# Batch 0 of a three-stage fp32 pipeline: three token tiles turned later, and unread products in the waits of the transform

## The reference, cut to what matters

```python
X = np.fft.fft(x, axis=1); X = np.fft.fft(X, axis=2)
u = x + np.real(X)                                   # x: (4, 768, 320)
mu = np.mean(u, axis=-1, keepdims=True)
var = np.mean((u - mu) ** 2, axis=-1, keepdims=True)
un = (u - mu) / np.sqrt(var + 1e-06)
out = u + np.maximum(un @ w_ch1, 0.0) @ w_ch2        # w_ch1: (320, 1280), w_ch2: (1280, 320)
```

## Time and profile before

| | |
|---|---|
| median of 3 runs | 972.84 us |
| lowest, highest | 966.74, 973.04 us |
| the profiled execution, its device time | 971.5 us |
| its span, first to last instruction | 969.7 us |
| mean granted PE clock | 0.935 |
| instructions | 29104 |
| PE busy in the span | 846.5 us (87%) |

### The profile page before, as it was taken

How to read it: one execution, slowest core, us unless ns; L and a number is a source line. 1 busy time by engine, 2 the same in 40 slices (tenths; PEclk the granted TensorE clock), 3 DMA queues, 4 the chain that set the end, 5 groups by cost and what they waited for, 6 DMA issues and landing times.

```text
span 969.7 us, 29104 instructions
## 1 busy us (share of the span) xinstructions
PE 846.5 (87%) x12612; PEld 810.1 (84%) x12612; DVE 595.4 (61%) x1187; ACT 386.8 (40%) x732; POOL 173.4 (18%) x191
## 2 busy tenths in 40 slices
PE   1738987997987997979879769999999999999998
PEld 1638876886886997978769669999999999999998
DVE  7692996785775685470446654776557573675622
ACT  1325315524424524525156334642446324562311
POOL 2016154182173074222100000000000000000000
PEclk9859997997997998996979979999999999999999
DMA  9601726476377186156682010000200001000000
GB/s 327 210 31 66 220 73 204 143 245 210 97 229 229 51 263 209 67 140 178 235 326 88 1 49 14 8 1 1 70 22 1 1 22 49 22 1 1 21 21 21
DMA packets 56095, 100.96 MB, mean 104 GB/s; under 512 B 28241, under 2 KB 40274, under 8 KB 51538
## 3 DMA queue, kind: packets, MB, share of 16 engines
q1 hardware_dynamic: 55970, 99.11, 31.0%
HBM read 76.40 MB, written 22.70 MB: 102 GB/s over the span
## 4 chain that ended last, share of the span: by engine, by line
PE 40%; DVE 8%; issue 1%; ACT 1%; DVEq 0%; POOL 0%; ACTq 0%
PE psum L1351 18%; PE psum L1411 9%; PE psum L1377 8%; PE psum L1431 2%; DVE stats L1234 1%; PE psum L1447 1%; DVE res L1244 1%; DVE hid L1180 1%; DVE res L1225 1%; DVE tok L1236 1%; PE psum L1342 1%; DVE cv L1257 1%; DVE res L1226 1%; DVE cv L1255 1%; DVE gs L1175 0%
## 5 line engine op out<-in xcount | busy, mean ns | idle before, releaser
L1351 PE MATMUL psum<-xn,w 128*128 128x384 f32 x640 | 126.6, 341 | 3.4 <-issue 3.4
L1351 PEld LDWEIGHTS psum<-xn,w 128*128 128x128 f32 x640 | 111.5, 190 | 4.4 <-issue 4.4
L1351 PE MATMUL psum<-xs,w 128*128 128x384 f32 x512 | 97.2, 343 | 10.2 <-PEq L1547 7.9
L1351 PEld LDWEIGHTS psum<-xs,w 128*128 128x128 f32 x512 | 91.6, 194 | 10.6 <-issue 10.6
L1377 PE MATMUL psum<-w,gs 128*128 128x320 f32 x576 | 89.9, 310 | 4.2 <-DVE gs L1175 4.1
L1377 PEld LDWEIGHTS psum<-w,gs 128*128 128x128 f32 x576 | 86.3, 188 | 5.7 <-DVE gs L1175 5.7
L552 DVE TENSOR_TENSOR score<-bank,mask 128x512 f32<-128x512 f32 x48 | 32.4, 688 | 71.0 <-PE bank L778 70.2
L535 DVE TENSOR_TENSOR inv<-inv,outer 128x31 f32<-128x31 f32 (+15 forms) x186 | 64.9, 349 | 6.4
L753 PE MATMUL bank<-inv_t,rhs 128*80 128x128 f32 x384 | 59.7, 329 | 9.2 <-POOL inv_t L452 4.6
L753 PEld LDWEIGHTS bank<-inv_t,rhs 128*80 128x80 f32 x384 | 56.2, 189 | 10.3 <-issue 9.8
L533 DVE TENSOR_TENSOR outer<-low,inv 128x31 f32<-128x31 f32 (+15 forms) x186 | 62.0, 334 | 4.3
(11 more groups left out here) (127 smaller groups left out, 1647.3 us busy)
## 6 DMA issues: line engine op xcount, KB each, us to landing
kb<-in_kb SPq DMA_DIRECT2D x24, 512.0 KB, 6.1
rt<-in_rt SPq DMA_DIRECT2D x12, 1024.0 KB, 7.2
w_in<-in_tables SPq DMA_DIRECT2D x13, 499.0 KB, 3.6
high_scratch<-w_in SPq DMA_DIRECT2D x13, 499.0 KB, 3.9
low_scratch<-w_in SPq DMA_DIRECT2D x13, 499.0 KB, 4.7
w_in<-in_w SPq DMA_DIRECT2D x6, 1040.5 KB, 5.1
at<-in_a SPq DMA_DIRECT2D x6, 1024.0 KB, 4.9
zt<-in_vt SPq DMA_DIRECT2D x12, 512.0 KB, 8.6
```

The source lines that it names most:

```text
L1351: last = mm(ps[bank][:, 0:HALF], a[:, 128 * f:128 * f + 128], y[:, HALF * half:HALF * (half + 1)], start=(i == 0), stop=(i == len(every) - 1))
```

## The change

For batch 0 alone, tiles 3 to 5 are turned after `second_up(d0, 2)`, and ACT's and DVE's instructions on them move with that, behind their work on `hidden` f = 2. On DVE, `centred` of tile 3 stays ahead of the three `turned_low`, tile 4 is centred behind them, and tile 5 and the variance sum behind `hidden_low(d0, 0)`. On PE `keep_busy` makes products of 384 columns from the first network's weights into a PSUM bank that nobody reads: 8 ahead of the spectrum (once that bank has been copied out), 7 ahead of each of the three turns, 8 ahead of `second_up(d0, 0)`; 37 in all. Batches 1 to 3 are as before.

```diff
# ACT
             hidden_high(d0, 0)
-            for t in range(FOLD, NT):
-                turned_high(b, t)
+            if b:
+                for t in range(FOLD, NT):
+                    turned_high(b, t)
             for f in range(1, 8):
                 hidden_high(d0, f)
+                if b == 0 and f == 2:
+                    for t in range(FOLD, NT):
+                        turned_high(b, t)
# DVE, batch 0
+                centred(b, FOLD)
+                for t in range(FOLD):
+                    turned_low(b, t)
+                centred(b, FOLD + 1)
+                hidden_low(d0, 0)
+                centred(b, FOLD + 2)
+                all_moments()
             for f in range(1, 8):
                 hidden_low(d0, f)
+                if b == 0 and f == 2:
+                    for t in range(FOLD, NT):
+                        turned_low(b, t)
# PE
+        def keep_busy(bank, n):
+
+            for i in range(n):
+                mm(ps[bank][:, 0:HALF], w1[:, 0, 0, 0:128], w1[:, 0, 0, 0:HALF], start=True, stop=True)
             first_down(b, NF - 1)
+            if b == 0:
+                pe.wait_ge(s_res, 1)
+                keep_busy(HALVES[0], 8)
             for t in range(FOLD):
+                if b == 0:
+                    keep_busy(HALVES[0], 7)
                 turn(b, t)
             if b == 0:
                 pe.wait_ge(s_w3, 48)
+                keep_busy(HALVES[0], 8)
             second_up(d0, 0)
-            for t in range(FOLD, NT):
-                turn(b, t)
+            if b:
+                for t in range(FOLD, NT):
+                    turn(b, t)
             for f in range(1, 8):
                 second_up(d0, f)
+                if b == 0 and f == 2:
+                    for t in range(FOLD, NT):
+                        turn(b, t)
                 second_down(d0, f - 1)
```

More of the change, by code:

```diff
@@ L1303, in _, with all_moments @@
                     hidden_low(d1, 5 + j)
-            for t in range(FOLD, NT):
[L1305 to L1310, removed]
-            if b:
+            def all_moments():
+                nc.vector.tensor_scalar(rstd[:, b % 2, :], moments[:, :, 1], 1e-6, None, ALU.add).then_inc(s_var, 1)
+            if b:
+                for t in range(FOLD, NT):
+                    centred(b, t)
+                    if t == FOLD + 1:
+                        hidden_low(d1, 8)
+                all_moments()
+                for t in range(FOLD):
+                    turned_low(b, t)
                 hidden_low(d1, 9)
                 result(d1)
-            hidden_low(d0, 0)
-            for t in range(FOLD, NT):
-                turned_low(b, t)
+                hidden_low(d0, 0)
+                for t in range(FOLD, NT):
+                    turned_low(b, t)
+            else:
+                centred(b, FOLD)
+                for t in range(FOLD):
+                    turned_low(b, t)
+                centred(b, FOLD + 1)
+                hidden_low(d0, 0)
+                centred(b, FOLD + 2)
+                all_moments()
             for f in range(1, 8):
                 hidden_low(d0, f)
+                if b == 0 and f == 2:
+                    for t in range(FOLD, NT):
+                        turned_low(b, t)
                 if f == 3:
```

## The result

The changed kernel took 967.26 us (median of 15 runs) against 973.04 us (15 runs) of the kernel before: ratio 0.9937, 95% interval 0.9909 to 0.9964. In a second comparison the ratio was 0.9961 (0.9928 to 0.9995). It is faster by 0.4 to 0.6%: less than 1%, but neither interval reaches 1. The forecast was 967, and "within 1%" at 0.90.

What follows compares the result with a forecast made beforehand. PE was taken as the bound, busy 87% of the span, so time saved before 571.50 comes off the end. Gains of 2.15, 1.12 and 1.50 sum to 4.77 us, forecasting 967 us, range 961.9 to about 971.8.

Steps and rivals of the forecast that it cites:

- The sum: Whole kernel: gains of 2.15, 1.12 and 1.50 us add to 4.77, giving 967 us; forecast's chance 0.62.
- Part 1, the order on DVE: DVE before `second_up(d0, 0)`: only tile 3 centred ahead, so the three `turned_low` start 2.15 us sooner, at no cost.
- starting near 564.9: Sign in the profile after: `second_up(d0, 0)` takes 1.40 us and starts near 564.9, before at 568.15.
- Part 2, ahead of the spectrum: Eight unread products on PE keep the clock up, so the spectrum's fold 2 ends 1.12 us sooner; 0 if it falls.
- Part 3, around the turns: Fillers around the turns hold PE's clock, so `second_up(d0, 0)` takes 1.40 us in place of 2.90: gain 1.50.
- The cover of 0.37 us: PE after tile 2: eight products fill to 564.51, `second_up(d0, 0)` due at 564.88, leaving 0.37 us.
- The spare of 0.4 us for ACT: Between `hidden_high` f = 2 and f = 3: ACT needs 3.6 us, PE is busy 3.99, leaving 0.4.
- the clock falls between the turns: Rival at the turns: PE's clock falls despite fillers, gain 1.7 us, total 969.8 or 970.5; chance 0.20.
- The late fillers: Rival at the turns: low-clock fillers and transposes take 3.44 us against 2.63 per tile, 2.5 us slower; chance 0.03.
- Dense fillers bring the clock back: Around the turns: argument against late fillers, that densely run unread products return PE to the high clock.
- The rows of batch 1: Rival: batch 1's row load comes late, margin shrinking from 4.4 to 0.3 us, 1.8 with idle time; chance 0.05.
- The larger gain: Rival: other executions lose more to the clock, 2 us more and up to run spread, 962 to 965; chance 0.10.

Runs made afterwards that it cites:

- the second pair: Second profiles of the unchanged earlier kernel and of the unchanged changed kernel; 51.25 and 46.80 us from batch 0's folding to batch 1's first product.
- order_only: Changed kernel without all 37 unread products; 50.20 us from batch 0's folding to batch 1's first product, total ratio 1.000 to the kernel before.
- no_spectrum_fill: Changed kernel without the eight unread products ahead of the spectrum; 51.02 us from batch 0's folding to batch 1's first product.
- fill_3: Changed kernel with 3 unread products ahead of each of the three turns in place of 7; 48.81 us from batch 0's folding to batch 1's first product.
- fill_14: Changed kernel with 14 unread products ahead of each of the three turns in place of 7; 47.83 us from batch 0's folding to batch 1's first product.
- transpose_fill: Changed kernel with identity transposes for the products around the turns (9 for 7, 10 for 8); 46.85 us from batch 0's folding to batch 1's first product.
- after_again: Changed kernel profiled once more, unchanged; 46.80 us from batch 0's folding to batch 1's first product, ratio 0.9961 to the kernel before.
- turns_f3: Changed kernel with tiles 3 to 5 turned one step later, behind `second_up(d0, 3)`; 47.23 us from batch 0's folding to batch 1's first product.
- after: Changed kernel, first profile; 46.86 us from batch 0's folding to batch 1's first product.
- turns_f1: Changed kernel, tiles 3 to 5 turned one step sooner, tile 5 centred ahead of `hidden_low(d0, 0)`; 46.74 us from batch 0's folding to batch 1's first product.
- network_fill: turns_f1 plus 36 unread products at the attention's end and 8 ahead of batch 0's third `first_up`; ratio 0.9915 to the kernel before.
- before: Kernel before the change, first profile; 51.09 us from batch 0's folding to batch 1's first product.
- before_again: Kernel before, profiled once more, unchanged; 51.25 us from batch 0's folding to batch 1's first product.
- fill_only: Kernel before, in its old order, with the 37 unread products added; 50.50 us from batch 0's folding to batch 1's first product, total ratio 0.9996.

## Why the prediction was right

**The sum.** Forecast 4.77 us, measured 4.23 in the stretch (4.45 between the second pair), and 5.8 between the medians of 15 runs with an interval of 3.5 to 8.9 (0.9964 and 0.9909 of 973.04). The second comparison gives 4.2 between the medians (973.39 and 969.23), with an interval of 0.5 to 7.0. The forecast of 967 met 967.26; with runs of before from 965.4 to 984.2 and of after from 959.9 to 970.3, that closeness is luck, and the 4.2 us of the stretch are the firmer number.

**Part 1, the order on DVE, 2.15 us.** The mechanism and the size of the earlier start are right: the start of `second_up(d0, 0)` moved by 2.83 us, of which 0.64 come from the spectrum, so 2.19. The sign "starting near 564.9" was missed by 0.44 (540.14 + 25.18 = 565.32), which is the shortfall of part 2. "Gain 2.15 us, cost nothing" was wrong as a price for the edit alone: order_only shows 0.89, because the clock stayed down just as long and more of the work fell into it. The terms of my sum were written as if they stood by themselves; they need each other.

**Part 2, ahead of the spectrum, 1.12 us.** Measured 0.64 (9.73 to 9.09), and the clock held. The term was mis-sized by 0.48: I took 0.184 us for each of fold 2's eight products. The three of L1437, with one row, and those between them take (541.60 - 540.14) / 5 = 0.29 us each at the full clock, so the five cost 0.54 us more than I gave them (the two groups ahead of them make up the rest, 0.12 more and 0.19 less). Before, these five had run at the full clock already, and there was nothing to win on them. no_spectrum_fill shows the other side: without the eight products that execution took 4.16 us more than the changed kernel.

**Part 3, around the turns, 1.50 us.** From the start of `second_up(d0, 0)` to the end of the stretch it was 23.08 us and is 21.68: 1.40. That is near the 1.50 with two errors that offset each other. The first two `second_up` went from 2.90 + 1.40 = 4.30 to 3.07, which is 1.23; and the nine transposes, which I had put at zero as unchanged, went from 1.26 to 0.98, since before they had begun at the low clock. The cover of 0.37 us behind the eight products was 0.17. The spare of 0.4 us for ACT ahead of `hidden_high` f = 3 was 0.47, and PE did not wait. Seven were enough, three were not (fill_3), fourteen delayed (fill_14).

**The rivals.** That the clock falls between the turns did not happen in any of the profiles with seven products, and the reason that the prediction took for it from the Trainium skill, in TensorE: Matmul & The Clock Gate, Part 4 (PE-mode transpose), that transposes don't count as PE activity in the way products do, fell with transpose_fill as far as holding the clock goes. The window that it named in support, 557.50 to 561.30, holds one group of three transposes and the first of the next, with 2.08 us of idle time between them, not two groups. The late fillers, 0.03, did not happen in the changed kernel, but are real: fill_3 shows them at the low clock, fill_14 at the high one. "Dense fillers bring the clock back" is no protection over so short a time: the eight of fill_3 ran slow for all of their 2.91 us. The rows of batch 1: predicted margin 0.3 us for ACT and 1.8 for PE; ACT was 1.54 us short of it (1.48 in after_again), as the load took 7.5 us to release it and not 5.7 (6.0 in turns_f3), and what was left for PE was about the 0.9 us by which the low part of f = 5 was ready ahead of `second_down`. The larger gain, from executions that lose more to the clock, has its mechanism shown in no_spectrum_fill, not its frequency.

**What stays open.** How often the kernel before runs the spectrum at the low clock for 10 us rather than 3.4. Of the four profiles with that wait unfilled one did, which is too few for a rate, so whether the mean gain is 4.2 us or nearer to the 5.8 of the first pair of medians is not settled. And why the attention ends between 472.6 and 488.3 us in the twelve profiles without a change in it; it is most of the spread of the totals and was not looked into.

## What to carry to other kernels

Two edits that each gained under a microsecond in their one profile gained four together, when one shortens a wait and the other keeps the clock over what is left: try them together before throwing either out. Filler has limits on both sides: it must reach from the last real work to close to the next, and it must end before the next is due at the clock at which it may come to run; ahead of each turn three were too few, seven right, fourteen too many. Three and fourteen have one profile each; of seven products, or nine transposes in their place, with the new order there are six (after, after_again, transpose_fill, turns_f3, turns_f1, network_fill), all between 46.74 and 47.23 us. And where a part that isn't touched varies by more than the change, measure from a mark behind it: the two profiles of the changed kernel agree to 0.06 us in the stretch and differ by 14 us in total.

## What the runs showed of the hardware

- The clock does not follow the work at once, in either direction. With the same idle time ahead (2.96 and 2.97 us), PE's first five spectrum products ran at 0.50 in the kernel before and at 1.00 in no_spectrum_fill; and behind the fall PE stayed at 0.50 for 3.4 us in the one and more than 10 us in the other while busy over 90% of the time.
- 128x128 fp32 transposes alone held the clock at 1.00 over 8.8 us in which PE was busy 5.98 us (transpose_fill, one profile).
- The row load of batch 1 is three transfers. The one of 768 KB landed 4.3 to 4.7 us after its issue in all profiles. The two of 192 KB behind it had a median of 4.9 to 5.1 us in those of before, before_again, order_only, fill_only, fill_14, turns_f1, turns_f3 and network_fill, and of 5.4 to 5.8 in those of after, after_again, no_spectrum_fill, transpose_fill and fill_3. Why is open; it took the margin that I had counted on.
- Products with a single row of weights (1x386) and the products between them took 0.29 us each on average at the full clock (five of them from 540.14 to 541.60 in the changed kernel), against 0.184 for a run of 128-row products of the same width.
